# 28 extra TensorE products of raw weights ahead of the first up product, in a recurrence followed by two gated layers

## The reference

```python
for t in range(S):
    state = alpha[:, :, t, :, None] * state + np.einsum('bhd,bhe->bhde', k[:, :, t], v[:, :, t])
    y[:, :, t] = np.einsum('bhd,bhde->bhe', q[:, :, t], state)
...
h = x @ w_in
g = h * (1.0 / (1.0 + np.exp(-1.702 * h)))
x = (g @ w_out)
...
h = x @ w_in
g = h - np.tanh(h)
return (g @ w_out)
```

## Time and profile before

| | us |
|---|---|
| median of 3 runs | 990.16 |
| the 3 runs | 988.91, 990.16, 993.03 |
| the profiled execution, its own time | 990.11 |
| its span, first to last instruction | 988.3 |
| TensorE busy | 954.0 (97% of the span) |
| VectorE, ScalarE, GpSimd busy | 535.0, 333.4, 275.9 |

### The profile page before, as it was taken

One profiled execution on the slowest core, in us unless ns is written; L12 is line 12 of the kernel. 1 busy time (PEld: TensorE's weight loads), 2 busy tenths in 40 slices (PEclk: granted clock), 3 DMA queues, 4 the chain that ended last, 5 costly groups with the idle time before them and its releaser, 6 DMA issues.

```text
span 988.3 us, 22169 instructions
## 1 busy us (share of the span) xinstructions
PE 954.0 (97%) x9312; PEld 823.5 (83%) x9312; DVE 535.0 (54%) x1349; ACT 333.4 (34%) x682; POOL 275.9 (28%) x314
## 2 busy tenths in 40 slices
PE   3698999999999999999999999999999999999997
PEld 3598999999999988888888888888888888888885
DVE  7679887778878867775421213434334333343332
ACT  1342233332332332323234544333233332333332
POOL 2554564646555554544000542000000000000000
PEclk9999999999999999999999999999999999999999
DMA  8633242333422422421023332020020010100100
GB/s 217 187 74 80 47 98 52 78 70 68 100 63 59 119 46 54 113 53 18 11 70 104 97 96 88 1 64 1 1 64 1 4 62 1 64 1 0 33 1 33
DMA packets 136501, 59.08 MB, mean 60 GB/s; under 512 B 114256, under 2 KB 131792, under 8 KB 136400
## 3 DMA queue, kind: packets, MB, share of 16 engines
q1 hardware_dynamic: 132672, 54.11, 21.9%
q10 hardware_dynamic: 3728, 3.54, 1.1%
HBM read 43.47 MB, written 14.16 MB: 58 GB/s over the span
## 4 chain that ended last, share of the span: by engine, by line
PE 94%; DMA 2%; DVE 2%; issue 1%; ACT 1%; SPq 0%; ACTq 0%; DVEq 0%
PE pX L710 38%; PE pZ L734 26%; PE pX L734 14%; PE pX L589 3%; PE pX L705 2%; PE pZ L616 2%; PE pZ L669 2%; PE pZ L625 2%; PE pZ L575 2%; PE pX L602 1%; PE pZ L660 1%; DMA x_raw<-attn_out 1%; DMA attn_out<-y 1%; DMA r<-q_t 0%; DVE r L1025 0%
## 5 line engine op out<-in xcount | busy, mean ns | idle before, releaser
L710 PE MATMUL pX<-x_hi,w_hi 128*128 128x512 f32 (+2 forms) x624 | 227.9, 365 | 0.7 <-ACT g L845 0.7
L710 PE MATMUL pX<-x_lo,w_hi 128*128 128x512 f32 (+2 forms) x624 | 227.5, 365 | 0.0
L710 PE MATMUL pX<-x_hi,w_lo 128*128 128x512 f32 (+2 forms) x624 | 227.4, 364 | 0.0
L1010 DVE TENSOR_TENSOR g_lo<-g,g_hi 128x512 fp32r<-128x512 f32 (+2 forms) x208 | 135.3, 650 | 159.9 <-ACT g_hi L850 159.8
L1109 DVE TENSOR_TENSOR g<-pX,sg 128x512 f32<-128x512 f32 x96 | 66.4, 691 | 177.6 <-ACT sg L847 177.6
L734 PE MATMUL pZ<-g_hi,w_hi 128*128 128x512 f32 (+2 forms) x416 | 151.8, 365 | 0.0
L734 PE MATMUL pZ<-g_lo,w_hi 128*128 128x512 f32 (+2 forms) x416 | 151.7, 365 | 0.0
L734 PE MATMUL pZ<-g_hi,w_lo 128*128 128x512 f32 (+2 forms) x416 | 151.6, 364 | 0.0
L850 ACT ACTIVATE g_hi<-g 128x512 fp32r<-128x512 f32 (+2 forms) x208 | 121.3, 583 | 78.1 <-DVE g L1109 74.5
L845 ACT ACTIVATE g<-pX 128x512 f32<-128x512 f32 (+3 forms) x144 | 65.7, 456 | 214.5 <-PE pX L710 179.1
L710 PEld LDWEIGHTS pX<-x_hi,w_hi 128*128 128x128 f32 x624 | 117.6, 188 | 17.8 <-ACT g L845 1.1
(11 more groups left out here) (75 smaller groups left out, 1114.1 us busy)
## 6 DMA issues: line engine op xcount, KB each, us to landing
v<-v_l SPq DMA_DIRECT2D x96, 48.0 KB, 2.4
x_raw<-hidden SPq DMA_DIRECT2D x6, 768.0 KB, 5.8
out_t<-o SPq DMA_DIRECT2D x12, 384.0 KB, 3.5
attn_out<-y SPq DMA_DIRECT2D x94, 48.0 KB, 1.9
alpha<-a_t SPq DMA_DIRECT2D x24, 128.0 KB, 3.0
r<-q_t SPq DMA_DIRECT2D x24, 128.0 KB, 3.0
k<-k_t SPq DMA_DIRECT2D x24, 128.0 KB, 3.0
w_raw<-w_in SPq DMA_DIRECT2D x16, 192.0 KB, 2.4
```

What stands on the lines that cost most here:

```text
L710: last = nc.tensor.matmul(pH(N)[:, 0:w], win(wp, f, m), XS[T % 2][xp][:, m, 0:w], start=(n == 0), stop=(n == len(terms) - 1))
L1010: nc.vector.tensor_tensor(GL[:, columns(N)], g_raw(N), GH[:, columns(N)].bitcast(F32), ALU.subtract).then_inc(gl_done, 1)
```

## The change

TensorE gets a function `warm_up`, called once, behind the state products of items 0 and 1 and ahead of the wait for state_step and of `up(0)`. It waits for the copy of item 0's outputs and for the first group of weights, then does 28 plain float32 products. Each multiplies columns 0 to 127 of a raw slice of w_in with columns 128 to 255 of the same slice, 128 x 128 by 128 x 128, into the first two quarters of the PSUM tensor pZ[0]. Nobody reads the results, and no semaphore is raised. Nothing is moved or taken out.

```diff
+            def warm_up(products):
+
+                pe.wait_ge(y_copied, 1)
+                pe.wait_ge(w_loaded[0][0], 16)
+                for n in range(products):
+                    nc.tensor.matmul(pZ[0][:, 0:2, 0:C], w_raw(0, n % 4)[:, 0:P], w_raw(0, n % 4)[:, P:2 * P].rearrange(
+                        "p (k t) -> p k t", k=2), start=True, stop=True)
+
...
                 state_products(j).then_inc(p_done, 1)
+            warm_up(28)
             pe.wait_ge(state_step, LEAD)
```

## The result

The changed kernel takes 986.26 us (median of 10 runs, 985.19 to 988.90) against 992.38 for the kernel before (10 runs on the same chip, 988.91 to 993.98). The ratio is 0.9945, with a 95% interval of 0.9931 to 0.9958: 0.55% faster, which is 5.5 us of 992.38, where the two medians differ by 6.1. The profiled execution took 986.29 us, of which 984.5 are the span; the one of before took 990.11.

A forecast was written before the change was run, and what follows sets the result against it. TensorE was taken to bound the kernel. Products ending at 32.36 plus a 5.91 us chain start up(3) at 38.27 instead of 41.48, 3.2 us earlier: 990.11 - 3.2 = 986.9 us, range 984.9 to 989.9.

The forecast's parts named there:

- What bounds the kernel, and the reading of the slow start: TensorE holds 94% of the chain, idles 7.8 us before up(0), and runs at 1.2 GHz until about 41.1 us.
- The cost of the products: In the gap before up(0): 28 products start at 23.87 and end at 32.36 us, 0.7 us behind x's arrival.
- the prediction's formula: End of the 28 products: 23.87 + 6.27 + 0.473 t, t being the time from their start to the clock's rise.
- The assumed 4.7: Time t in us from the new products' start to the clock's rise, taken as the middle of bounds 0 and 9.4.
- The chain behind them: up(0) to up(3) takes 5.91 us instead of 9.79; VectorE and GpSimd hold nothing up, with 1.5 us slack.
- Whether the gain reaches the end: The stop at 94.7 us before block 2 comes 3.2 us sooner, stays 3.4 us long, and the gain stays.
- the term of before: The slow stretch from up(0) to up(3) in the kernel before, put at 9.79 us from one profile.
- The bounds of t: Clock rise 0 to 9.4 us after the new products' start: gain 3.88 to 1.0 us, time 986.2 to 989.1.
- The fall behind the second stop: Rival: the 1.2 GHz stretch at 99.14 us, after the stop at 94.7, goes too; 1.7 us gained, 985.2; chance 0.14.
- the time is lost at the stop: Before block 2, x's load has its own date, so a longer stop returns all 3.2 us; 990.1; chance 0.07.
- the clock falls again in the mixed stretch: Behind up(0), small products and a ScalarE stop return TensorE to 1.2 GHz; 0.7 us later, 990.8; chance 0.05.
- the products don't raise the clock: The 28 take 11.9 us, end at 35.8, and all behind stays slow; 4.1 us later, 994.2; chance 0.04.

The follow-up runs named there:

- first filler kernel: Changed kernel plus 12 unread 128x128 products in the second stop, ahead of the up product at N = 28: 986.08 us, ratio 0.9946.
- behind x: Changed kernel with its 28 products also waiting for x, so they stand on the path instead of in the gap: 993.91 us, ratio 1.0041.
- before, again: The kernel before, unedited, timed and profiled once more: 990.74 us, ratio 1.0005; the profiled execution took 989.54 us.
- before with the filler: Kernel before plus 12 unread 128x128 products ahead of the up product at N = 28, none at the start: 990.29 us, ratio 0.9987.
- earlier x alone: Kernel before with unit 0's stores and the first x load issued ahead of unit 2's q and k loads, no extra products: 989.41 us, ratio 0.9984.
- small products: Changed kernel with 56 products of 48 rows by 64 columns by 64 in place of its 28 of 128x128: 996.50 us, ratio 1.0048.
- changed again: The changed kernel, unedited, on the chip of the last comparison: 985.58 us, ratio 0.9948; the profiled execution took 988.33 us.
- 14 with the earlier x: Kernel before with 14 products and unit 0's stores and first x load ahead of unit 2's q and k loads: 984.07 us, ratio 0.9929.

## Why the prediction was right, and where it was not

**What bounds the kernel, and the reading of the slow start.** Right. The printed 1.00 ahead of the first record was an absent record: profiles that have a record there show 0.50 (18.1 to 38.6, 19.8 to 47.1).

**The cost of the products.** Right. They took 8.19 us against a forecast of 8.5, started 0.5 us sooner because the prelude did, and ended at 31.5 instead of 32.4. In the four profiles with 28 of them in a row they take 8.19, 9.21, 8.37 and 8.36 us. The changed kernel's rise came 3.5 us after their start; in the profile of the first filler kernel the 28 took 9.21 us, which by the prediction's formula is a rise 6 us after. The assumed 4.7 lies between. The second 28 of the 56 products confirm the price at full pace: all 56 hold `up(0)` back by 38.59 - 24.24 = 14.35 us, the 28 behind x by 8.20, so 28 more cost 6.15 us in the traces, forecast 6.3; the runs give 6.5 to 7.0.

**The chain behind them.** `up(0)` to `up(3)` took 37.73 - 31.72 = 6.0 us, forecast 5.9. VectorE and GpSimd held nothing up.

**Whether the gain reaches the end.** Right in kind. `up(3)` is 3.75 us sooner in the profiled pair, and the execution 3.8 us shorter. The second stop moved with TensorE and was 2.7 us long, where the prediction kept it at 3.4; that 0.6 us was lost again behind it (890.8 us from the end of the stop to the end, against 890.2).

**What failed is the term of before.** The prediction took 9.79 us from one profile for the slow stretch, and wrote that "that execution lies 0.05 us from the median, so the same number stands for it". It was the median of three runs. Over 85 runs before lies between 988.0 and 994.3 with a median of 991.1, and the largest of the things that vary is how long the start stays slow. From the start of `up(0)` to that of item 3's state products (the second L602 behind it, L604 in the kernels with the earlier x) the profiles give:

| profile | slow until | start of up(0) | item 3's L602 | us |
|---|---|---|---|---|
| changed kernel | (never) | 31.72 | 41.53 | 9.8 |
| before, again | 38.6 | 31.14 | 44.03 | 12.9 |
| before | 41.1 | 31.69 | 45.28 | 13.6 |
| before with the filler | 47.1 | 31.83 | 47.52 | 15.7 |
| earlier x alone | 45.5 | 28.88 | 44.67 | 15.8 |
| 14 products | 49.6 | 32.68 | 48.47 | 15.8 |
| small products | 51.6 | 35.55 | 51.37 | 15.8 |

So the benefit is 3.1, 3.8, 5.9 or 6.0 us by execution. Only two of these six slow starts are the kernel before itself, and they give the two small values, so how often each length comes isn't known. But the 5.1 and 6.1 us between the medians of the two comparisons (5.2 and 5.5 by the ratios) lie in that span, while the forecast had taken one of the low ones, less 0.7 us for products that outlast the gap. The bounds of t covered a late rise within the new products, but the same uncertainty was left out of the chain that they replace, where it is larger: there TensorE stops for 0.37 to 0.45 us again and again, and the rise came up to 17 us after `up(0)`.

Two other things vary too, in both kernels. x arrives by chance sooner or later: where its load isn't moved ahead and no product holds it back, `up(0)` starts between 31.1 and 32.8 us. And the clock falls or stays behind the second stop, 2.0 us as worked out below. In between, from item 3's L602 to the end of the second stop, all eleven profiles with that stop unfilled take 52.0 to 53.0 us. The slow execution with 14 products, 994.36 against the 990.11 of before, is put together so: 1.0 us of later x, 2.2 of longer slow start, 1.3 behind the second stop, less 0.2 in between. The changed kernel takes away the slow start alone; its own runs still spread over 4 us.

**The forecast of the time** was close because two errors cancelled: the execution that it started from, 990.1 us, was 2.3 us under before's median in that comparison (1.0 under that of all 85 runs), and the gain was put 2.9 us (or 1.9) too low. Of the chances, "faster by over 0.5%" had 0.09. The measured 0.55% (0.42 to 0.69) and 0.52% lie on that border, so whether it came true isn't settled, but 0.09 was too low, for the same reason. That the time fell in the range is in part luck.

**The rivals.** The fall behind the second stop is indeed a matter of the single execution. Eleven profiles have that stop unfilled, 2.5 to 3.4 us long. The clock fell in six of them (before, before again, changed, changed again, 14 products, the earlier x alone) and not in five (56 products, behind x, small ones, 14 with the earlier x, 22). With the fall of 3.4 us, the time from the end of the stop to the end of the span is 890.2, 890.8, 891.3, 891.5 and 891.5 us; without, 888.6, 888.7, 889.0, 889.2 and 889.6. The price is 2.0 us between the two means, forecast 1.7. With the fall of 6.8 us (the earlier x alone) it is 891.8. The rival that the time is lost at the stop, and the one that the clock falls again in the mixed stretch, didn't happen in any profile. The rival that the products don't raise the clock didn't happen with these products, and did with the small ones, with the price that it named: slower than before.

**What stays open.** What the clock did in the five longer executions with 22 products, whether the filler one step later would bring the 2 us, and why like stops leave the clock up in one execution and bring it down in another.

## What to carry to other kernels

Where TensorE waits several microseconds for a transfer and its next products run at half pace, fill the wait up to the arrival with full-size products that nobody reads: too few leave a stop in which the clock can fall again (14: no gain; 22: five of ten runs as slow as before), and too many cost their full time. Shortening the wait is worth its own time on top, and needs fewer products. Before pricing such a change from one profile, look at the spread of the runs: a spread of several microseconds in the kernel before can mean that the profile shows one of several lengths of the slow stretch, and then the term needs a range too.

## What the runs showed of the hardware

In these profiles TensorE's clock rose late and unevenly when its products had short stops: with full-size products back to back the pace doubled within 3 to 6 us, while with the up products, mixed with small ones and with stops of 0.37 and 0.45 us, it rose between 7 and 17 us after the first. The same stop of 2.5 to 3.4 us brought the clock down in six of eleven profiles. And 112 records of 48x64 products, 12.2 us without a stop, left the clock at 1.2 GHz, at 0.109 us each, half of the 0.22 us of a 128x128 record at that clock; yet the recurrence's own small products are followed by a stretch at full clock up to 18.1 in one profile. So "small products don't raise the clock" holds for those of the experiment and isn't a rule; what sets the two kinds apart wasn't tested.
